# Attention values by column groups of two heads, with rotary, maxima and inverse sums placed elsewhere

## The chip, the core and the metric

One core of a Trainium2 chip runs the whole program in one launch. The metric is the time of an execution in microseconds (us) on the device. TensorE (PE in the rows) multiplies, VectorE is DVE, ScalarE is ACT, GpSimd is POOL, and SyncE (SP) issues the transfers. The engines run their own queues in order and meet at semaphores.

## What is computed

```python
q_rot, k_rot = rotate(q), rotate(k)                # 4 batches x 8 heads, 576 positions, 64 wide
scores = q_rot @ k_rot.T / 8
attn = exp(scores - rowmax(scores)); attn /= attn.sum(-1) + 1e-9
x = concat_heads(attn @ v)                         # 2304 tokens x 512
h = x @ w_in;  x = (h - tanh(h)) @ w_out           # 512 -> 2048 -> 512
h = x @ w_in2; out = (h * sigmoid(1.702 h)) @ w_out2
```

All of it is float32. The kernel keeps that precision in the scores and in the two expert layers by cutting an operand into a high part in the rounded format fp32r and a low rest, and multiplying the parts; probabilities times V is a plain float32 product.

## The kernel before, in words

The first part is attention, head by head, 32 heads in 16 pairs (heads 2p and 2p+1 share the 128 partitions of a load). A head has TILES = 5 tiles of 128 rows; 576 = 4*128 + 64. For each head:

- `load` (line 199) brings k and q transposed, and a copy with the halves exchanged (`turned`); `rope` on VectorE (line 656) turns them with three operations for k and three for q, for a pair at once.
- `keys_hi`, `queries_hi` on ScalarE (lines 547, 553) make the high parts; SyncE copies them to the other half of the partitions (`copy_k`, `copy_q`, lines 217, 221); `keys_lo`, `queries_lo` on VectorE (lines 677, 682) make the low rests. This runs PREPARED = 3 heads ahead in 4 sets of buffers.
- "M" tiles: `near_scores` (line 406) gives scores good enough for the row maxima, with queries on the partitions; `row_max` on VectorE (line 665) reduces each tile to a column. Then "R": `maxima_across` (line 418) transposes the five columns, and `place_maxima` (line 670, VectorE, one operation with a mask) writes them as rows into `q_max`.
- "S" tiles: `scores` (line 423) gives scores minus maxima with keys on the partitions, in four multiplications; `exp` on ScalarE (line 532) writes `probs`; `probs_v` (line 441) multiplies two tiles behind (PV_LAG). Its weights are `v_one`, 64 columns of V beside 64 columns of ones, so that the sums of the probabilities fall out in the other 64 partitions. It makes two multiplications of 288 columns a tile.
- `copy_pv` on ScalarE (line 540) empties the accumulator; the sums go through SyncE to `invert` on VectorE (line 688), through memory and back as `inv_wide`, GpSimd multiplies (`normalise`, line 375), and `store_x` writes the head pair to memory.

M, R and S tiles take turns in three slots of two PSUM banks each, in the order that `ring_order` (line 46) writes out by hand. The tile at place i waits in `slot_free` (line 393) until the reader of the tile at place i-3 is done: `exp` for S, `row_max` for M, `place_maxima` for R.

The second part, two expert layers of 6 units of 384 tokens, runs over 16 slices of the hidden width: `first_product` (line 471), tanh or sigmoid on ScalarE, a product or difference on VectorE, cut again, `second_product` (line 489). Tokens are fetched and cut a unit ahead (`load_x`, `cut_x`, from slice CUT_AT = 8 on); for the first unit this is done during attention (`early_x`), as are the first weights (`early_w`).

Of the kernel before, what the change touches and what calls it, by code (L numbers as in the profile page):

```python
# [40 lines left out]
PROBS = 5  # L41
PV_LAG = 2
PREPARED = 3


def ring_order():

    order = []
    for h in range(-2, NHEADS):
        now, ahead = h >= 0, 0 <= h + 1 < NHEADS  # L50
        for t in range(TILES):
            if now:
                order.append(("S", h, t))
            if ahead and t < 2:
                order += [("M", h + 1, 2 * t + 1), ("M", h + 1, 2 * t + 2)]
            if ahead and t == 2:
                order.append(("R", h + 1, 0))
        if h + 2 < NHEADS:
            order.append(("M", h + 2, 0))
    return order  # L60
# [5 lines left out]
def program(nc, q, k, v, w_in1, w_out1, w_in2, w_out2, cos_t, sin_t, out):  # L66
    q_d, k_d = (t.rearrange("b h d s -> (b h d) s") for t in (q, k))
    v_d = v.rearrange("b h s d -> (b h) s d")
    x_scratch = [nc.dram_tensor(f"x_scratch{m}", [DM, TOKENS], F32, kind="Internal").ap() for m in range(LAYERS)]
    inv_scratch = nc.dram_tensor("inv_scratch", [PAIRS, 2, SEQ], F32, kind="Internal").ap()  # L70
# [3 lines left out]
    with ExitStack() as ctx:  # L74
# [8 lines left out]
        pv_banks = PS[:, 6:8, 0:HALF]  # L83
# [9 lines left out]
        tile_mask = g_raw[0:TILES, :, :].rearrange("p a n -> p (a n)")[:, 0:PADDED].rearrange("p (t n) -> p t n", t=TILES)  # L93
        g_hi = sb("g_hi", [P, STAGES, UNIT], F32R)
        g_lo = sb("g_lo", [P, STAGES, UNIT], F32R)
        y_sb = sb("y_sb", [P, KC, BANK])
        w_parts = [sb(f"w_parts{j}", [P, 4, BANK], F32R) for j in range(APART)]
# [8 lines left out]
        k_one = [sb(f"k_one{j}", [P, PADDED], F32R, one_stack) for j in range(4)]  # L106
        q_hh = [sb(f"q_hh{j}", [P, PADDED], F32R, one_stack) for j in range(4)]
        q_max = [sb(f"q_max{j}", [P, PADDED], F32R, one_stack) for j in range(4)]
        v_one = [sb(f"v_one{j}", [P, 2, TILES, P], stack=one_stack) for j in range(2)]
        probs = [sb(f"probs{j}", [P, SEQ], stack=one_stack) for j in range(PROBS)]  # L110
# [3 lines left out]
        pv_sb = [sb(f"pv_sb{j}", [P, SEQ], stack=one_stack) for j in range(4)]  # L114
        sums = [sb(f"sums{j}", [P, 2 * SEQ // P], stack=one_stack) for j in range(2)]
        inv_wide = [sb(f"inv_wide{j}", [P, SEQ], stack=one_stack) for j in range(2)]
        x_out = [sb(f"x_out{j}", [P, SEQ], stack=one_stack) for j in range(2)]
# [8 lines left out]
        v_ready_to_load = sem("v_ready_to_load")  # L126
# [50 lines left out]
        def slot_columns(slot, cols):  # L177
            return slot.rearrange("p b n -> p (b n)")[:, 0:cols]
# [19 lines left out]
        def _(sp):  # L198
# [85 lines left out]
            for h in range(-1, NHEADS):  # L284
# [19 lines left out]
                if h == 12:  # L304
                    load_x(0, 0)
# [508 lines left out]
```

## Time and profile before

| | |
|---|---|
| median of 3 runs | 1148.81 us (1148.41 to 1148.97) |
| the profiled execution, its own time | 1147.27 us |
| its span in the trace | 1145.5 us, so 1.8 us lie around it |
| mean granted clock of TensorE | 0.997 |
| busy TensorE / VectorE / ScalarE / GpSimd | 1104.1 / 552.4 / 425.7 / 57.1 us |

A matmul's record starts when it is taken up and ends when its last result is modelled to have left, so records overlap: the distance between starts tells what the array needs, the length of a record doesn't. A plain float32 multiplication leaves two records, each with its own weight load; one on fp32r leaves one.

### The profile page before, as it was taken

What the parts mean: (1) busy time and instruction counts of PE and PEld (TensorE: products, weight loads), DVE (VectorE), ACT (ScalarE), POOL (GpSimd) and SP (SyncE); (2) the same over time, 40 slices, a digit from 0 to 9 for tenths busy, and PEclk for the clock granted to TensorE, in tenths of its full rate; (3) what the DMA queues carried; (4) which work ended last, traced back from release to release, by engine and by line L of the source; (5) the groups of instructions that cost most, each with busy time, mean ns of one, the idle gap of its engine ahead of it and who ended that gap; (6) DMA issues with size and microseconds to landing.
All of it is one profiled execution on the core that took longest, in us unless ns stands there. A gap on an engine that the chain in (4) does not pass through costs nothing.

```text
span 1145.5 us, 15078 instructions
## 1 busy us (share of the span) xinstructions
PE 1104.1 (96%) x5952; PEld 1017.8 (89%) x5952; DVE 552.4 (48%) x879; ACT 425.7 (37%) x747; POOL 57.1 (5%) x62
## 2 busy tenths in 40 slices
PE   2999998999999999999999999999999999999998
PEld 1888877787789999999999999999999999999997
DVE  7888887888736433232233333455232322323222
ACT  2555554555544423222222323445232222323222
POOL 3011111102111000000000000000000000000000
PEclk9999999999999999999999999999999999999999
DMA  6355557566315300000000100062000000000000
GB/s 182 95 158 127 155 154 201 136 169 166 87 61 178 102 28 29 28 28 11 19 28 28 29 28 28 1 193 83 28 28 28 28 1 28 28 28 1 28 1 28
DMA packets 78854, 79.85 MB, mean 70 GB/s; under 512 B 30144, under 2 KB 55744, under 8 KB 78784
## 3 DMA queue, kind: packets, MB, share of 16 engines
q1 hardware_dynamic: 78784, 78.89, 24.1%
q8 instruction: 47, 0.77, 0.3%
q14 instruction: 23, 0.19, 0.1%
HBM read 55.12 MB, written 14.23 MB: 61 GB/s over the span
## 4 chain that ended last, share of the span: by engine, by line
PE 89%; DVE 7%; SPq 1%; DMA 1%; POOL 1%; issue 1%; ACT 0%; POOLq 0%; DVEq 0%; ACTq 0%
PE PS L485 35%; PE PS L503 17%; PE PS L500 17%; PE PS L449 10%; PE PS L414 3%; PE PS L431 3%; PE PS L437 3%; DVE neg_max L667 2%; DVE q_max L684 1%; DVE k_hl L679 1%; DVE q_max L674 1%; DMA turned_k<-k_dram 1%; DVE raw_q L662 0%; DVE w_parts L697 0%; DVE raw_q L660 0%
## 5 line engine op out<-in xcount | busy, mean ns | idle before, releaser
L485 PE MATMUL PS<-x_hi,w_parts 128*128 128x384 f32 x1536 | 423.1, 336 | 0.0
L742 DVE TENSOR_TENSOR g_raw<-PS,act_t 128x384 f32<-128x384 f32 x192 | 107.0, 557 | 400.2 <-ACT act_t L610 202.1
L485 PEld LDWEIGHTS PS<-x_hi,w_parts 128*128 128x128 f32 x1536 | 280.5, 188 | 4.3
L485 PE MATMUL PS<-x_lo,w_parts 128*128 128x384 f32 x768 | 257.2, 335 | 0.0
L500 PE MATMUL PS<-g_hi,w_parts 128*128 128x384 f32 x768 | 210.3, 334 | 0.8 <-DVE g_lo L747 0.8
L503 PE MATMUL PS<-w_parts,g_hi 128*128 128x512 f32 x576 | 195.1, 393 | 1.0 <-DVE y_sb L756 0.8
L449 PE MATMUL PS<-probs,v_one 128*128 128x288 f32 x640 | 183.4, 409 | 0.3 <-ACT pv_sb L545 0.3
L747 DVE TENSOR_TENSOR g_lo<-g_raw,g_hi 128x384 fp32r<-128x384 f32 x192 | 107.7, 561 | 113.6 <-ACT g_hi L617 113.6
L537 ACT ACTIVATE probs<-PS 128x576 f32<-128x576 f32 x160 | 104.0, 650 | 129.6 <-PE PS L437 126.3
L485 PEld LDWEIGHTS PS<-x_lo,w_parts 128*128 128x128 f32 x768 | 144.2, 188 | 4.2
L617 ACT ACTIVATE g_hi<-g_raw 128x384 fp32r<-128x384 f32 x192 | 100.8, 525 | 122.9 <-DVE g_raw L742 119.7
L500 PEld LDWEIGHTS PS<-g_hi,w_parts 128*128 128x128 f32 x768 | 140.0, 188 | 1.1 <-DVE g_lo L747 1.1
L449 PEld LDWEIGHTS PS<-probs,v_one 128*128 128x128 f32 x640 | 112.4, 191 | 18.1 <-issue 0.5
L667 DVE TENSOR_REDUCE neg_max<-PS 128x1 f32<-128x576 f32 x160 | 113.8, 746 | 30.1 <-PE PS L414 29.5
L500 PE MATMUL PS<-g_lo,w_parts 128*128 128x384 f32 x384 | 128.3, 334 | 0.0
L503 PEld LDWEIGHTS PS<-w_parts,g_hi 128*128 128x128 f32 x576 | 108.1, 188 | 21.9 <-issue 1.1
L610 ACT ACTIVATE act_t<-PS 128x384 f32<-128x384 f32 x96 | 47.2, 492 | 212.5 <-PE PS L485 212.5
L608 ACT ACTIVATE act_t<-PS 128x384 f32<-128x384 f32 x96 | 47.2, 492 | 206.9 <-PE PS L485 206.9
L414 PE MATMUL PS<-k_hl,q_hh 128*128 128x288 f32 x320 | 86.7, 376 | 34.8 <-DMA q_hh<-q_hh 17.5
L503 PE MATMUL PS<-w_parts,g_lo 128*128 128x512 f32 x288 | 113.7, 395 | 0.0
L414 PEld LDWEIGHTS PS<-k_hl,q_hh 128*128 128x128 f32 x320 | 56.4, 200 | 51.8 <-issue 19.7
L431 PE MATMUL PS<-q_hh,k_hl 128*128 128x288 f32 x320 | 80.0, 332 | 0.0
(51 smaller groups left out, 741.3 us busy)
## 6 DMA issues: line engine op xcount, KB each, us to landing
x_raw<-x_scratch SPq DMA_DIRECT2D x12, 768.0 KB, 4.5
raw_w<-moe_w_in_dram SPq DMA_DIRECT2D x32, 256.0 KB, 3.1
raw_w<-moe_w_out_dram SPq DMA_DIRECT2D x32, 256.0 KB, 3.3
raw_k<-k_dram SPq DMA_DIRECT2D x16, 288.0 KB, 3.5
turned_k<-k_dram SPq DMA_DIRECT2D x64, 72.0 KB, 3.2
raw_q<-q_dram SPq DMA_DIRECT2D x16, 288.0 KB, 3.8
turned_q<-q_dram SPq DMA_DIRECT2D x64, 72.0 KB, 3.5
k_one<-k_hl SPq DMA_DIRECT2D x32, 144.0 KB, 2.4
```

Source lines behind the costliest of these rows:

```text
L414: last = nc.tensor.matmul(slot[:, b, :], q_hh[h % 4][:, t * P:(t + 1) * P], k_hl[h % 4][:, b * HALF:(b + 1) * HALF], start=True, stop=True)
L431: nc.tensor.matmul(slot[:, b, :], k_hl[h % 4][:, keys], q_hh[h % 4][:, b * HALF:(b + 1) * HALF], start=True, stop=False)
L449: last = nc.tensor.matmul(pv_banks[:, b, :], v_one[h // 2 % 2][:, h % 2, t, :], probs[g % PROBS][:, b * HALF:(b + 1) * HALF], start=t == 0 ...
L485: last = nc.tensor.matmul(h_banks[j % 2], w_parts[j][:, w, c * P:(c + 1) * P], x[par][:, c, :], start=(c == 0 and w == 0 and x is x_hi), s ...
L500: last = nc.tensor.matmul(acc_banks[c][:, 0:UNIT], w_parts[j][:, w, c * P:(c + 1) * P], g[:, s, :], start=start, stop=stop)
L503: last = nc.tensor.matmul(acc_banks[c], g[:, s, c * P:(c + 1) * P], w_parts[j][:, w, :], start=start, stop=stop)
L537: nc.scalar.activation(probs[g % PROBS][:, :].rearrange("p (b n) -> p b n", b=2), slot_halves(slot_of("S", h, t)), ACT.Exp).then_inc(exp_d ...
L608: nc.scalar.activation(act_t[:, j % 2, :], h_banks[j % 2], ACT.Tanh).then_inc(act_done, 1)
L617: nc.scalar.activation(g_hi[:, j % STAGES, :], g_raw[:, j % 2, :], ACT.Copy).then_inc(g_hi_done, 1)
L667: nc.vector.tensor_reduce(neg_max[h % 2][:, t:t + 1], slot_halves(slot_of("M", h, t)), AX.XY, ALU.max, negate=True).then_inc(max_done, 1)
L742: nc.vector.tensor_tensor(g_raw[:, j % 2, :], h_banks[j % 2], act_t[:, j % 2, :], ALU.subtract if m == 0 else ALU.mult).then_inc(g_done, 1)
L747: nc.vector.tensor_tensor(g_lo[:, j % STAGES, :], g_raw[:, j % 2, :], g_hi[:, j % STAGES, :].bitcast(F32), ALU.subtract).then_inc(g_lo_don ...
```

## The change

Attention goes pair by pair. A new schedule (`near_plan`, `near_tiles`, `pair_steps`) interleaves the two heads tile by tile, with the ten M tiles of the next pair between. One step of TensorE is: S of the even head; at the fifth step the two transposes R of the next pair; the first M tiles of the step; `values` of the step before; S of the odd head; the second M tiles. `values` replaces `probs_v`: V of the even head stands in the array's columns 0 to 63 and V of the odd head in 64 to 127, each fed by its own probabilities, 512 columns and then 64; the sums are made by four multiplications with 32 columns of ones, one in each quarter of the columns. The other edits: rotary runs on VectorE for pair 0 and from pair 3 on, and on GpSimd for pairs 1 and 2; ScalarE places the maxima, in five operations a head, each with a column of the identity as its scale; there are 6 sets of keys and queries instead of 4; V is laid out by the host in tiles, one transfer a pair; the accumulator is emptied by three copies a pair; GpSimd no longer normalises, the values are stored unscaled, and the inverse sums are fetched a unit at a time and multiplied in by VectorE before the tokens are cut in the first layer (`scale_x`).

```diff
@@ schedule @@
-PROBS = 5
-PV_LAG = 2
-PREPARED = 3
+PROBS = 6
+SETS = 6
+UNITS_PV = PAIRS * TILES
+def near_plan(pair):
+    if pair == 0:
+        return [(0, 0), (0, 2), (2, 2), (2, 2), (0, 0)]
+    return [(1, 2), (1, 2), (1, 2), (1, 0), (0, 0)]
+def near_tiles(pair):
+    return [(2 * pair + i % 2, i // 2) for i in range(2 * TILES)]
 def ring_order():
+    order = [("M", h, t) for h, t in near_tiles(0)] + [("R", 0, 0)]
+    for pair in range(PAIRS):
+        for n, (first, second) in enumerate(pair_steps(pair)):
+            order.append(("S", 2 * pair, n))
+            if n == TILES - 1 and pair + 1 < PAIRS:
+                order.append(("R", 2 * pair + 2, 0))
+            order += [("M", h, t) for h, t in first]
+            order.append(("S", 2 * pair + 1, n))
+            order += [("M", h, t) for h, t in second]
+        def score_count(h, t):
+            return h // 2 * 2 * TILES + 2 * t + h % 2 + 1
-        early_x = {17: (0, 1), 19: (2, 3)}
-        early_w = {21: 0, 23: 1, 25: 2, 27: 3, 31: 4}
+        early_x = {8: (0, 1), 9: (2, 3)}
+        early_w = {10: 0, 11: 1, 12: 2, 13: 3, 15: 4}
@@ SyncE @@
+            def fetch_sums(pair):
+                sp.wait_ge(pv_copied, pair + 1)
...
+                for g in range(4):
+                    sp.dma_start(sums[pair % 2][32 * g:32 * g + 32, :],
+                                 sum_sb[pair % 2][32 * g:32 * g + 1, :].rearrange("o (p j) -> o p j", p=32)).then_inc(sums_in[pair % 2], 16)
+                if m == 0:
...
+                    for a in range(2):
+                        rows = inv_scratch.rearrange("c a n -> a c n")[a:a + 1, :, u * UNIT:(u + 1) * UNIT]
+                        sp.dma_start(inverses[own(a), :, :], rows.broadcast_to([HD, KC, UNIT])).then_inc(inverses_in, 16)
+            for pair in range(PAIRS):
+                if pair:
+                    fetch_sums(pair - 1)
+                    store_x(pair - 1)
+                if pair + 2 < PAIRS:
+                    copy_k(2 * pair + 4)
+                    copy_q(2 * pair + 4)
+                if pair + 1 < PAIRS:
+                    load_v(pair + 1)
+                if pair + 2 < PAIRS:
+                    copy_k(2 * pair + 5)
+                    copy_q(2 * pair + 5)
+                if pair:
+                    store_inverse(pair - 1)
+                if pair + 4 < PAIRS:
+                    for t, src in (("k", k_d), ("q", q_d)):
+                        sp.wait_ge(k_lo_done if t == "k" else q_lo_done, 2 * pair + 6)
+                        load(t, src, pair + 4)
@@ TensorE @@
                 else:
-                    pe.wait_ge(row_done, h + 1)
+                    pe.wait_ge(row_done, h + 2)
-            def probs_v(g):
...
+            def values(unit):
+                pair, t = divmod(unit, TILES)
+                pe.wait_ge(exp_done, 2 * unit + 2)
+                if t == 0:
+                    pe.wait_ge(loaded["v"][pair % 2], pair // 2 * 16 + 16)
+                    if pair:
+                        pe.wait_ge(pv_copied, pair)
+                first, last = t == 0, t == TILES - 1
+                p = [probs[(2 * unit + a) % PROBS] for a in range(2)]
+                for bank, cols in ((values_wide, slice(0, BANK)), (values_tail, slice(BANK, SEQ))):
+                    for a in range(2):
+                        nc.tensor.matmul(bank[own(a), :], v_sb[pair % 2][:, t, own(a)], p[a][:, cols],
+                                         start=first, stop=last, skip_group_check=True)
+                for g in range(4):
+                    done = nc.tensor.matmul(sum_rows[32 * g:32 * g + 32, :], ones[:, t // FULL, :],
+                                            p[g // 2][:, g % 2 * HALF:(g % 2 + 1) * HALF], start=False, stop=last,
+                                            skip_group_check=True)
+                done.then_inc(pv_done, 1)
@@ ScalarE @@
+            def copy_pv(pair):
...
+                nc.scalar.activation(pv_sb[pair % 2][:, 0:BANK], values_wide, ACT.Copy)
+                nc.scalar.activation(pv_sb[pair % 2][:, BANK:SEQ], values_tail, ACT.Copy)
...
+                nc.scalar.activation(sum_sb[pair % 2][:, :], sum_rows, ACT.Copy).then_inc(pv_copied, 1)
+            def place_maxima(h):
+                act.wait_ge(r_ready, h + 1)
+                for t in range(TILES):
+                    last = nc.scalar.activation(q_max[h % SETS][max_rows(h % 2), t * P:(t + 1) * P],
+                                                slot_of("R", h - h % 2)[0:TILES, h % 2, 0:P], ACT.Copy, scale=ident[0:TILES, t:t + 1])
+                last.then_inc(row_done, 1)
+                for n in range(TILES):
+                    exp(2 * pair, n)
+                    if n == 0 and pair:
+                        copy_pv(pair - 1)
+                    if n == TILES - 1 and pair + 1 < PAIRS:
+                        place_maxima(2 * pair + 2)
+                    exp(2 * pair + 1, n)
+                    if n == TILES - 1 and pair + 1 < PAIRS:
+                        place_maxima(2 * pair + 3)
...
+                    elif b < NHEADS:
+                        if n == 1:
+                            keys_hi(a)
+                            queries_hi(a)
+                        if n == 2:
+                            keys_hi(b)
+                        if n == 3:
+                            queries_hi(b)
@@ VectorE, for pairs from 1 on (a, b = 2 * pair + 4, 2 * pair + 5) @@
+                    for h, t in first:
+                        row_max(h, t)
...
+                        if n == 1 and pair + 3 < PAIRS:
+                            rope("k", pair + 3)
+                        if n == 2:
+                            split(a)
+                        if n == 3:
+                            split(b)
+                        if n == 4 and pair + 3 < PAIRS:
+                            rope("q", pair + 3)
+                    if n == 3 and pair:
+                        invert(pair - 1)
+                    for h, t in second:
+                        row_max(h, t)
...
+            def scale_x(u, chunks=range(KC)):
+                dve.wait_ge(x_loaded, u * 16 + 16)
+                dve.wait_ge(inverses_in, u * 32 + 32)
+                for c in chunks:
+                    nc.vector.tensor_tensor(x_raw[:, c, :], x_raw[:, c, :], inverses[:, c, :], ALU.mult).then_inc(x_scaled, 1)
@@ GpSimd @@
-            for pair in range(PAIRS - 1):
-                normalise(pair)
-            normalise(PAIRS - 1)
+            pool.wait_ge(q_lo_done, 2)
+            for pair in (1, 2):
+                rope("k", pair)
+                rope("q", pair)
```

## Rows read from the trace of the kernel before

**Rows 1.** The page: span, busy time of each engine.
```profile
span 1145.5 us, 15078 instructions
PE 1104.1 (96%) x5952; PEld 1017.8 (89%) x5952; DVE 552.4 (48%) x879; ACT 425.7 (37%) x747; POOL 57.1 (5%) x62
```

**Rows 2.** Stretches: start:end length, busy us (records) of PE, PEld, DVE, ACT, POOL, clock, DMA share, GB/s.
```profile
40.00:150.00 110.00, 109.78 (x618) 93.57 (x616) 96.48 (x145) 63.27 (x97) 14.06 (x10) 1.00 0.54 140
150.00:170.00 20.00, 18.15 (x103) 15.20 (x102) 18.11 (x24) 10.17 (x16) 3.77 (x2) 1.00 0.62 166
170.00:190.00 20.00, 17.99 (x102) 15.12 (x101) 15.74 (x21) 10.04 (x16) 3.51 (x2) 1.00 0.74 203
190.00:210.00 20.00, 17.59 (x88) 14.16 (x87) 16.37 (x24) 10.60 (x17) 2.83 (x2) 0.91 0.62 156
210.00:290.00 80.00, 75.76 (x420) 63.78 (x419) 70.90 (x106) 45.37 (x70) 11.51 (x8) 1.00 0.60 160
290.00:310.00 20.00, 17.59 (x91) 14.89 (x90) 14.93 (x19) 9.84 (x16) 3.90 (x2) 0.91 0.32 87
...
400.00:500.00 100.00, 100.00 (x579) 100.00 (x578) 30.53 (x56) 27.84 (x56) 0.00 (x0) 1.00 0.07 24
```

**Rows 3.** The chain between 160 and 180 us, its last piece.
```profile
176.30 6.15 DMA turned_k<-k_dram
```

**Rows 4.** Groups between 95 and 149 us, three head pairs long.
```profile
L449 PE MATMUL PS<-probs,v_one 128*128 128x288 f32 x119 | 33.8, 406 | 0.0
L667 DVE TENSOR_REDUCE neg_max<-PS 128x1 f32<-128x576 f32 x30 | 21.5, 746 | 5.0 <-PE PS L414 4.9
L537 ACT ACTIVATE probs<-PS 128x576 f32<-128x576 f32 x30 | 19.5, 651 | 21.2 <-PE PS L437 20.3
...
L382 POOL TENSOR_TENSOR x_out<-pv_sb,inv_wide 64x576 f32<-64x576 f32 x6 | 8.4, 1405 | 46.2 <-DMA inv_wide<-inv_scratch 46.0
L674 DVE TENSOR_TENSOR q_max<-PS,g_raw 5x640 fp32r<-5x640 f32 x6 | 4.9, 810 | 0.1
```

**Rows 5.** TensorE in order of time, 160 to 163 us: start, length, records.
```profile
160.13 1.14 PE L449 MATMUL PS<-probs,v_one 128*128 128x288 f32 x4
161.10 0.27 PE L421 MATMUL PS<-ident,neg_max 128*5 128x128 f32 x1
161.13 0.51 PE L431 MATMUL PS<-q_hh,k_hl 128*128 128x288 f32 x2
161.48 0.43 PE L437 MATMUL PS<-q_max,k_one 69*128 69x288 f32 x2
161.74 1.13 PE L449 MATMUL PS<-probs,v_one 128*128 128x288 f32 x4
```

**Rows 6.** A multiplication's end and the exponential behind it; ScalarE back to back.
```profile
108.38 0.43 PE L437 MATMUL PS<-q_max,k_one 69*128 69x288 f32 x2
...
108.84 0.65 ACT L537 ACTIVATE probs<-PS 128x576 f32<-128x576 f32 x1
...
257.74 0.63 ACT L537 ACTIVATE probs<-PS 128x576 f32<-128x576 f32 x1
...
258.27 0.67 ACT L557 ACTIVATE q_hh<-raw_q 64x576 fp32r<-64x576 f32 x1
...
258.84 0.63 ACT L537 ACTIVATE probs<-PS 128x576 f32<-128x576 f32 x1
```

**Rows 7.** Groups of ScalarE over the whole span, by width.
```profile
L625 ACT ACTIVATE y_sb<-PS 128x512 f32<-128x512 f32 x10 | 5.4, 596 | 2.2 <-PE PS L503 2.2
L625 ACT ACTIVATE y_sb<-PS 128x384 f32<-128x384 f32 x12 | 5.2, 488 | 2.2 <-PE PS L500 2.2
...
L583 ACT ACTIVATE warm<-ident 128x1 f32<-128x1 f32 x1 | 0.2, 203 | 0.0
```

**Rows 8.** The start: first near scores, first maxima, first transpose, first scores.
```profile
17.46 1.78 PE L414 MATMUL PS<-k_hl,q_hh 128*128 128x288 f32 x6 [17.46 <-DMA q_hh<-q_hh]
...
19.49 3.42 DVE L667 TENSOR_REDUCE neg_max<-PS 128x1 f32<-128x576 f32 x5
...
23.82 0.68 PE L431 MATMUL PS<-q_hh,k_hl 128*128 128x288 f32 x2
```

**Rows 9.** Groups of VectorE in the expert layers.
```profile
L742 DVE TENSOR_TENSOR g_raw<-PS,act_t 128x384 f32<-128x384 f32 x192 | 107.0, 557 | 400.2 <-ACT act_t L610 202.1 <-ACT act_t L608 198.1
...
L703 DVE TENSOR_TENSOR x_lo<-x_raw,x_hi 128x384 fp32r<-128x384 f32 x48 | 23.6, 553 | 0.1
```

More of the change, by code:

```diff
@@ new lines, in _ @@
+            for h in range(2, 4):
+                copy_k(h)
+                copy_q(h)
+            for t, src in (("k", k_d), ("q", q_d)):
+                sp.wait_ge(k_lo_done if t == "k" else q_lo_done, 4)
+                load(t, src, 3)
+            for pair in range(PAIRS):
[13 more added lines that the diff above has]
+                if pair + 4 < PAIRS:
+                    for t, src in (("k", k_d), ("q", q_d)):
+                        sp.wait_ge(k_lo_done if t == "k" else q_lo_done, 2 * pair + 6)
+                        load(t, src, pair + 4)
+                if pair == 6:
@@ new lines, in _ @@
+            maxima_across(0)
+            for pair in range(PAIRS):
+                for n, (first, second) in enumerate(pair_steps(pair)):
+                    scores(2 * pair, n)
+                    if n == TILES - 1 and pair + 1 < PAIRS:
+                        maxima_across(pair + 1)
+                    for h, t in first:
+                        near_scores(h, t)
+                    if pair * TILES + n:
+                        values(pair * TILES + n - 1)
+                    scores(2 * pair + 1, n)
+                    for h, t in second:
+                        near_scores(h, t)
@@ L520, in unit @@
                 second_product(m, u, FC - 1)
[L522 removed]
             first_product(0, 0, 0, 0)
[L524 removed]
+            values(UNITS_PV - 1)
             first_product(0, 0, 0, 1)
@@ L704, in cut_x @@
                                             ALU.subtract).then_inc(x_lo_done, 1)
-            for j in range(4):
+            nc.vector.memset(ones[:, 0, :], 1.0)
+            nc.vector.memset(ones[0:TAIL, 1, :], 1.0)
+            nc.vector.memset(ones[TAIL:P, 1, :], 0.0)
+            for j in range(SETS):
                 dve.wait_ge(cleared, j + 1)
-                last = nc.vector.memset(k_one[j][max_rows(j % 2), :].bitcast(F32), 1.0)
+                last = nc.vector.memset(k_one[j][max_rows(j % 2), 0:SEQ].bitcast(F32), 1.0)
@@ L796, in rope_tables, with value_tiles @@
     return [np.concatenate([t, t], 0) for t in tables]
+def value_tiles(v):
+    t = np.zeros((PAIRS, PADDED, 2, HD), np.float32)
+    t[:, 0:SEQ] = v.reshape(PAIRS, 2, SEQ, HD).transpose(0, 2, 1, 3)
+    return t.reshape(PAIRS, TILES, P, P).transpose(0, 2, 1, 3)
 def kernel(**inputs):
```

409 lines of the change are left out of this document (181 added, 228 removed).

## The prediction, made before the changed kernel ran

> **What bounds the kernel now.** I read the page first: TensorE is busy for 1104.1 of 1145.5 us, VectorE for 552.4 [rows 1]. The share is an average over two parts, so I read stretches next. In the expert layers TensorE has no gap at all and VectorE works 30.5 us of 100 [rows 2]: nothing that the change does there can shorten it, and only the edit on VectorE could lengthen it. In attention TensorE is busy for 109.78 of 110 us between 40 and 150 us, with VectorE at 96.48 and ScalarE at 63.27 [rows 2]. From 150 to 310 us it loses time: 1.85, 2.01 and 2.41 us in three stretches of 20, 4.24 us in the 80 behind them, 2.41 us in the last, together 12.9 us, and twice the granted clock reads 0.91, one dip to the 1.2 GHz level each [rows 2]. The longest single piece is a wait of 6.15 us for a load of keys that stands behind eight transfers of weights on SyncE's queue [rows 3].
>
> The groups between 95 and 149 us give the price of a head pair: 60 probabilities-times-V multiplications in 119 found records (120 are due), 30 maxima and 30 exponentials are three pairs, so a pair takes 54 / 3 = 18.0 us [rows 4].
>
> **What `values` costs on TensorE.** The four records of a tile of `probs_v` last 1.14 us together and one lasts 0.406 [rows 4, 5], so starts are (1.14 - 0.406) / 3 = 0.24 us apart for 288 columns, and a tile costs 0.97 us, a tile of both heads 1.94. A record of 512 columns is then 512 / 288 * 0.242 = 0.43 us, one of 64 columns 0.05. Records double, 16 for 8 a pair tile. No row shows two multiplications in different column groups at once, so I bound it. All one after the other: 4 * 0.43 + 4 * 0.05 + 8 * 0.242 = 3.9 us. Groups fully side by side: 2 * 0.43 + 2 * 0.05 + 2 * 0.242 = 1.45 us. The nearest rows are those of narrow weights between wide ones: the transpose with 5 columns starts at 161.10, exactly four intervals of 0.24 behind 160.13; the second record of L431 must start one interval of 0.13 before L437 at 161.48, so its first one began to stream at about 161.22. The narrow one cost 0.12 us, though its own record is 0.27 long [rows 5]: narrow weights enter and leave with the work around them in flight. That speaks for an array that takes instructions of another column range as it goes, and I take 1.45 us, plus 0.05 for hand-overs (their bound is the 0.15 us by which a record outlasts its interval). That is 1.50 for 1.94, -0.44 us a pair tile, -2.2 us a pair. Without the hand-overs a pair has 18.0 - 2.5 = 15.5 us of TensorE work.
>
> **What the new order adds.** Before, TensorE hardly waits in the steady stretch. To see whether it will, I walk through a pair with durations from rows. S costs 4 * 0.131 = 0.53 us, an M tile 0.26. An exponential starts 0.2 us after its last multiplication stopped streaming, since its record outlasts the interval by 0.16 and 0.03 more pass [rows 6], lasts 0.65 [rows 4], and the waiting multiplication streams about 0.16 later, with its weights still to load.
> (a) Slot of the transposes. The first M tile of a pair stands three places behind R, so it waits until both heads' maxima are placed. From the end of S of the even head's fifth tile TensorE has 0.22 (transposes) + 1.45 + 0.53 + 0.53 = 2.7 us to do. ScalarE can start the odd head's exponential 0.2 us behind that S, at 2.4, issues the five narrow copies behind it at 3.0 and is done at 4.05. ScalarE's 1, 384 and 512 columns last 203, 488 and 596 ns [rows 7], so 128 columns last 0.28; back to back ScalarE starts 0.53 to 0.57 us apart what lasts 0.63 to 0.67 [rows 6], so the narrow ones come every 0.20 us. With 0.16 to restart: a wait of 1.5 us.
> (b) Behind `values` of the old pair ScalarE makes three copies of 512, 64 and 288 columns, 1.0 us, ahead of the exponential of the odd head's first tile. The next S needs that slot: 0.2 + 1.0 + 0.65 + 0.16 = 2.0 us, against 1.05 us of work (S and two M): a wait of 1.0 us.
> (c) At the third and fourth tile, S of the even head needs the slot of the odd head's S before it, with only two M between: 0.2 + 0.65 + 0.16 - 0.53 = 0.5 us, twice.
> (d) An M tile waits for a maximum that stands behind the three operations of the keys' rotary on VectorE, and `values` once for an exponential behind the splitting on ScalarE: 0.4 and 0.3 us.
> Together 4.2 us a pair. A pair takes 15.5 + 4.2 = 19.7 us in place of 18.0: +1.7 * 16 = +27 us, and the hand-overs add 0.05 * 80 = +4.
>
> **What goes.** The 12.9 us of late waits [rows 2]. Copies now run two pairs ahead in 6 sets and loads of keys a pair ahead, so a burst of weights, 6.15 us late at its worst, has some 16 us of cover; the early cutting of tokens and weights falls into time that VectorE now has: 16.7 us a pair before, less two placements of 0.81 [rows 4], is 15 of 19.7. I take all 12.9; without that cover they stay.
>
> **The start.** Ten M tiles must be reduced before the first S instead of five. The first maximum starts 2.03 us behind the first multiplication at 17.46, five take 3.42 us [rows 8], so ten end at about 26.3, and with transposes and placing S starts near 28, not 23.8. Four M tiles of 0.26 are only moved here, and the next pair's are done sooner: net +2 us. GpSimd turns pairs 1 and 2 in 12 operations; its nearest row is 1.4 us for 64 partitions [rows 4], so 17 us, until about 33 us. Pair 1 is asked for at 30, pair 2 much later; up to 4 us of stall here go into the range.
>
> **At nothing.** 32 multiplications of GpSimd (1.4 us each) waited for transfers all the time [rows 4] and nobody near waited for them. SyncE issues 21 transfers a pair where it had 24 (V one for four, sums four for two, no inverses out) and 2 a unit in the first layer. `scale_x` adds four operations of 0.55 us a unit [rows 9] at the ninth slice, so VectorE and, behind it, ScalarE are held for about 4.5 us with the cutting; the next slice's g is then ready some 0.3 us before TensorE asks, and if it isn't, the cost is under 0.5 us for each of five units.
>
> **Sum.** 1147.3 (profiled execution) + 27 + 4 + 2 - 12.9 = 1167. That execution lies 1.5 us below the median of 1148.8, so I forecast 1168 us.
>
> **Rivals.**
> 1. *Short waits, faster.* If (a) to (d) come to less than (16 * 2.5 + 12.9 - 2 - 4) / 16 = 2.9 us a pair, the kernel is faster. The place is ScalarE's queue at the pair change: with narrow copies every 0.1 us, copies of the accumulator in 0.6, and exponentials picked up while M tiles last, (a) is 0.8, (b) 0.6, (c) and (d) 0.7, together 2.1: 1168 - 16 * 2.1 = 1134. For it: in the rows short operations are the least certain, and ScalarE idles 21.2 us before 30 exponentials [rows 4]. Against it: 0.2 us is what one column alone takes.
> 2. *Groups in file.* The two halves of a float32 multiplication use the same columns, so the low half waits for the high one, and if TensorE begins records strictly in order the next group can only run beside the low half. V then takes 3 * 0.43 + 2 * 0.05, the sums 5 * 0.242: 2.6 us, +0.67 on 1.94; waits as before but for (d), 3.7: 1147.3 + 80 * 0.67 + 16 * 3.7 + 2 - 12.9 = 1249, 1251 for the median. For it: every record in the rows starts behind the one ahead of it. The Trainium skill, "TensorE: Matmul & The Clock Gate", The mechanism, says that matmuls keep program order in start and end; the rows agree, and whether a pending half blocks the next group is not in them.
> 3. *No side by side at all.* 3.9 us a pair tile: + 80 * 1.93 instead of 0.67, so 1352. For it: nothing but that no row shows an overlap.
> 4. *Drains.* Each pair tile goes from 128-column weights to 64, to 32 and back. If each passage let the array run empty, 0.16 us by which a record outlasts its interval, it would be 3 * 0.16 * 80 = 38 us: 1168 - 4 + 38 = 1202. The transpose in [rows 5] cost 0.12 us with both its passages, which speaks against it. The Trainium skill, "TensorEngine Tiling (Array Packing)", Key Properties, states that a change of tiling mode drains TensorE; by that rule the sum is this rival's, and the trace disagrees as far as it shows such a change.
>
> **Chances.** Forecast 0.35, rival 1 0.27, rival 2 0.20, rival 3 0.10, rival 4 0.08. A measurement of this kernel tells some 0.2% (2.3 us) from no change. Of rival 1 and of the forecast's lower edge 0.05 fall within it: faster 0.25, same 0.05, slower 0.70. The range goes from 1130 (waits of 2 us a pair) to 1260 (rival 2 with some stalls of the start) and leaves out rival 3 and some edges. The forecast's own range is 1150 to 1190.
>
> **What would show it.** Records of `values`: starts of the two heads' wide multiplications nearly together and a pair tile in 1.5 us (2.6 in file, 3.9 one by one, 1.9 with drains). The distance of pairs 19.7 us with TensorE's waits for the placed maxima (1.5) and for exponentials (1.0, 0.5, 0.5). No wait for keys near 176 us. ScalarE's narrow copies 0.28 us long and 0.20 apart. The expert layers unchanged to 2 us. The forecast is wrong if the pair tile isn't near 1.5 us, or if ScalarE doesn't hold TensorE at the pair change.

## The result, and the profile after

The changed kernel takes 1204.41 us (median of four runs, 1202.62 to 1205.79), the kernel before 1148.66 beside it (1148.41 to 1148.97): ratio 1.048, 95% interval [1.0466, 1.0502]. It is slower by 55.7 us. The forecast was 1168, so sign and range held, but the loss is nearly three times the +19 that was forecast. The profiled execution of the changed kernel took 1203.67 us, 56.4 more than that of before.

The page of the changed kernel, against [rows 1]:

```profile
span 1201.9 us, 16365 instructions
PE 1133.3 (94%) x6592; PEld 959.0 (80%) x6592; DVE 527.8 (44%) x860; ACT 457.0 (38%) x923; POOL 26.1 (2%) x42
```

TensorE stays the busiest, but is now idle for 1201.9 - 1133.3 = 69 us where it was for 41. Stretches of the changed kernel, columns as in [rows 2]:

```profile
40.00:150.00 110.00, 96.09 (x678) 58.07 (x670) 72.57 (x107) 59.97 (x132) 0.00 (x0) 0.95 0.45 112
150.00:310.00 160.00, 141.62 (x991) 82.97 (x990) 108.20 (x164) 89.54 (x195) 0.00 (x0) 0.95 0.56 135
...
450.00:550.00 100.00, 100.00 (x579) 100.00 (x578) 32.30 (x60) 28.07 (x57) 0.00 (x0) 1.00 0.12 35
```

In attention TensorE waits for 13.9 of 110 us where it waited for 0.2; the expert layers are full again. The first multiplication of the experts begins at 390.64 us instead of 337.05, +53.6; the other 2.8 come behind it.

Where the 53.6 lie is read from the transposes, one pair of which stands in every head pair. The distances from one pair's to the next, worked out from their starts:

```
before: 18.3 18.2 18.2 18.2 18.2 18.2 18.2 20.3 24.4 20.1 19.5 19.5 19.5 22.5 18.2
after:  22.3 26.4 21.5 21.5 22.6 21.5 21.5 22.9 22.4 22.3 23.8 24.0 24.0 24.0 24.0
```

Three stages: the first two distances lose 12.2 us, the next five 17.4 (a steady pair takes 21.46 instead of 18.2), the last eight 23.3, although before had its own losses there.

**The pair tile.** TensorE in order of time, the stretch that answers to [rows 5]:

```profile
158.37 0.42 PE L428 MATMUL PS<-k_hl,q_hh 128*128 128x288 f32 x2
158.73 1.19 PE L469 MATMUL PS<-probs,v_sb 128*64 128x512 f32 x8
159.85 0.69 PE L473 MATMUL PS<-probs,ones 128*32 128x288 f32 x8
160.47 0.53 PE L447 MATMUL PS<-g_lo,g_hi 128*128 128x288 f32 x2
```

Eight records with 64 columns of V and eight of ones, then S. The single records of that stretch, start in us and distance to the record ahead in ns:

```
158.503  132  M,    128 columns of weights, 288 streamed
158.726  223  V,    64 columns, 512 streamed, even head, high half
158.733    7  V,    the odd head's
159.206  473  V,    even head, low half
159.212    6  V,    the odd head's
159.636  424  V,    64 streamed, high half (then 6, 49, 6)
159.849  152  ones, 32 columns, 288 streamed (then 7, 6, 8)
160.116  246  ones, low half (then 7, 7, 6)
160.471  335  S,    128 columns, 288 streamed, first record
160.712  241  S,    second record
160.843  131  M-part of S
```

Two things are to be seen. First, the column groups run fully side by side: records of different groups start 6 to 8 ns apart, also where the low halves wait for the high ones. Second, each change of the weights' width leaves a gap. M's last record owes 0.131, V starts 0.092 behind that and its first record takes 0.473 + 0.007 where 0.427 would do: 0.145 us for 128 to 64 columns. By the same working, always from a group's record to its own next one, 64 to 32 costs 0.13 (0.105, and 0.027 in the first record), and 32 to 128 costs 0.22 (0.115 before S's first record, 0.11 within it). Together 0.50 us. A pair tile takes 158.634 to 160.581, 1.95 us, and took 1.94: the columns saved 0.49 and the passages took 0.50. The expectations below were written with 0.12 to 0.20 a passage and 0.46 a tile, which leaves out part of the 7 ns steps between groups.

Two more readings tell what kind of gap this is. Where S stood still for an exponential, its first two records start at 174.908 and 175.146, 0.24 us apart as behind the sums, and not 0.13 as elsewhere: behind a passage TensorE starts up as it does behind a wait. And the change between float32 and fp32r isn't the cause: in the kernel before, V is followed by S at one width, V's last record at 98.895 and S's second at 99.270, which is 0.375 us for the 0.242 + 0.131 that they owe. The length of such a pair of records says nothing of a gap, since the first is taken up early; in the kernel before, S directly behind V is

```profile
162.50 0.64 PE L431 MATMUL PS<-q_hh,k_hl 128*128 128x288 f32 x2
```

**The pair change.** The timeline of ScalarE, with TensorE beside it, where the next pair's maxima are placed:

```profile
183.09 0.38 PE L437 MATMUL PS<-ident,neg_max 128*5 128x128 f32 x2
...
184.14 0.65 ACT L561 ACTIVATE probs<-PS 128x576 f32<-128x576 f32 x1
...
184.82 1.36 ACT L578 ACTIVATE q_max<-PS,ident 5x128 fp32r<-5x128 f32 x5
...
186.20 0.65 ACT L561 ACTIVATE y_sb<-PS 128x576 f32<-128x576 f32 x1
...
186.32 0.50 PE L453 MATMUL PS<-q_max,k_one 69*128 69x288 f32 x2
...
186.75 1.34 ACT L578 ACTIVATE q_max<-PS,ident 5x128 fp32r<-5x128 f32 x5
187.99 0.62 ACT L561 ACTIVATE y_sb<-PS 128x576 f32<-128x576 f32 x1
...
188.14 0.53 PE L428 MATMUL PS<-g_hi,g_lo 128*128 128x288 f32 x2 [1.32 <-ACT q_max L578]
```

The transposes are made at 183.1, their slot is free at 188.1: the ten narrow copies take 1.36 and 1.34 us and each set stands behind an exponential. The waits between 97 and 183 us, four pairs long (total, times, longest):

```profile
PEld PS L469 <- issue: 14.0, 55, 0.5
PEld PS L447 <- issue: 7.9, 16, 0.9
...
PE PS L428 <- ACT q_max L578: 5.3, 4, 1.3
PEld PS L447 <- ACT y_sb L561: 4.6, 10, 0.7
PEld PS L447 <- ACT probs L561: 3.1, 6, 0.7
```

Against the list of the prediction, per pair and measured from end of stream to next start: (a) 1.58 us (said 1.5), (b) 0.70 (1.0), (c) 0.48 twice (0.5 twice), (d) nothing (0.7), and 0.29 for the first S, which waits for its own placed maxima (not foreseen). Together 3.5 us, where 4.2 were forecast.

**The late pairs.** Stretches at and behind one pair change of the changed kernel, columns as in [rows 2]:

```profile
252.00:257.00 5.00, 2.82 (x24) 1.72 (x20) 3.88 (x8) 4.95 (x15) 0.00 (x0) 0.99 0.60 65
257.00:260.40 3.40, 3.40 (x18) 1.08 (x17) 0.76 (x1) 0.04 (x1) 0.00 (x0) 0.51 0.99 288
```

At the change ScalarE is full (4.95 of 5 us) and TensorE half idle (2.82 of 5); right behind it the granted clock is 0.51, the 1.2 GHz level, for 3.4 us, in which up to 1.7 us of work are lost. ScalarE's queue at such a change:

```profile
274.84 0.68 ACT L602 ACTIVATE q_hh<-raw_q 64x576 fp32r<-64x576 f32 x1
275.54 1.06 ACT L618 ACTIVATE w_parts<-raw_w 128x1024 fp32r<-128x1024 f32 x1
276.51 0.64 ACT L561 ACTIVATE probs<-PS 128x576 f32<-128x576 f32 x1
277.17 1.35 ACT L578 ACTIVATE q_max<-PS,ident 5x128 fp32r<-5x128 f32 x5
```

The cutting of expert weights (1.06 us) now stands ahead of the exponential and the maxima. From the eleventh distance on a pair takes 23.8 to 24.0 us: 21.46, some 0.8 of more waiting (the tenth distance, which has no dip, takes 22.3), and up to 1.7 of clock. There are nine such dips in attention, the first of them, at 55.5 us, twice as long as the others; before had two.

**The start.** The 26.4 us at the second distance are one wait of 4.4 us: TensorE's first M tile of pair 2 starts at 55.98. GpSimd was long done (its last rotary operation starts at 33.52 and lasts 1.80). ScalarE's and SyncE's rows show who was late:

```profile
51.67 1.34 ACT L578 ACTIVATE q_max<-PS,ident 5x128 fp32r<-5x128 f32 x5
52.91 0.67 ACT L602 ACTIVATE g_lo<-raw_q 64x576 fp32r<-64x576 f32 x1
...
53.60 0.47 SPq L242 DMA_DIRECT2D g_lo<-g_lo  x1
...
55.98 0.82 PE L428 MATMUL PS<-g_hi,g_lo 128*128 128x288 f32 x2 [4.37 <-issue]
```

The queries' high part is cut behind the narrow copies, then copied by a transfer that is issued at 53.60 and that the multiplication needs. The narrow copies are not all of it: with the maxima on VectorE (a run below) TensorE still waits 3.1 us there, until 57.73. The cut of the queries then stands behind an exponential that itself waits for its scores until 54.11.

**The expert layers.** TensorE where the first ones begin:

```profile
398.02 0.44 PE L525 MATMUL PS<-g_hi,w_parts 128*128 128x384 f32 x1 [0.95 <-DVE g_lo L844]
...
437.19 0.44 PE L525 MATMUL PS<-g_hi,w_parts 128*128 128x384 f32 x1 [0.98 <-DVE g_lo L844]
```

One gap of 0.95 us at the hand-over from attention, one of 0.98 behind the ninth slice with `scale_x` in it, and one of 0.20: 2.1 us, where before had a single gap of 0.78 at its hand-over. Another 1.1 of the +2.8 is attention's: its last pair tile, with both heads, stands behind the experts' first slice and takes up 2.0 us there, where before had one head's, 0.9. The rest is in small pieces.

### The profile page after: what moved, and what is told of

Its sections match the earlier page's. It is cut to its first block, busy times and chain, and to the rows that moved or that the text cites. A ratio compares the mean times of both kernels' runs of the same rounds, so it can differ in the third digit from the quotient of the medians.

```text
span 1201.9 us, 16365 instructions
## 1 busy us (share of the span) xinstructions
PE 1133.3 (94%) x6592; PEld 959.0 (80%) x6592; DVE 527.8 (44%) x860; ACT 457.0 (38%) x923; POOL 26.1 (2%) x42
## 4 chain that ended last, share of the span: by engine, by line
PE 84%; ACT 8%; issue 3%; DVE 3%; POOL 1%; DMA 0%; SPq 0%; ACTq 0%; POOLq 0%; DVEq 0%
PE PS L510 33%; PE PS L528 16%; PE PS L525 16%; PE PS L469 7%; PE PS L447 4%; PE PS L473 4%; ACT q_max L578 3%; PE PS L453 2%; ACT y_sb L561 2%; PE PS L428 2%; ACT probs L561 1%; DVE neg_max L736 1%; ACT q_hh L602 1%; ACT w_parts L618 1%; POOL q_max L386 0%
## 5 line engine op out<-in xcount | busy, mean ns | idle before, releaser
L561 ACT ACTIVATE y_sb<-PS 128x576 f32<-128x576 f32 x79 | 51.1, 649 | 76.8 <-PE PS L453 76.5
L453 PE MATMUL PS<-q_max,k_one 69*128 69x288 f32 (+1 forms) x320 | 71.2, 305 | 6.7 <-ACT q_max L578 6.3
L428 PE MATMUL PS<-k_hl,q_hh 128*128 128x288 f32 x220 | 46.8, 325 | 30.9 <-DMA q_hh<-q_hh 17.9
L469 PE MATMUL PS<-probs,v_sb 128*64 128x512 f32 (+1 forms) x324 | 71.6, 455 | 0.8 <-ACT probs L561 0.6
L525 PEld LDWEIGHTS PS<-g_lo,w_parts 128*128 128x128 f32 x384 | 72.1, 188 | 0.0
L561 ACT ACTIVATE probs<-PS 128x576 f32<-128x576 f32 x81 | 52.1, 645 | 46.6 <-PE PS L453 46.3
```

The costliest lines, as they stand in the source:

```text
L428: last = nc.tensor.matmul(slot[:, b, :], q_hh[h % SETS][:, t * P:(t + 1) * P], k_hl[h % SETS][:, b * HALF:(b + 1) * HALF], start=True, sto ...
L453: last = nc.tensor.matmul(slot[:, b, :], k_one[h % SETS][rows, keys], q_max[h % SETS][rows, b * HALF:(b + 1) * HALF], start=False, stop=True)
L469: nc.tensor.matmul(bank[own(a), :], v_sb[pair % 2][:, t, own(a)], p[a][:, cols], start=first, stop=last, skip_group_check=True)
L525: last = nc.tensor.matmul(acc_banks[c][:, 0:UNIT], w_parts[j][:, w, c * P:(c + 1) * P], g[:, s, :], start=start, stop=stop)
L561: nc.scalar.activation(probs[i % PROBS].rearrange("p (b n) -> p b n", b=2), slot_halves(slot_of("S", h, t)), ACT.Exp).then_inc(exp_done, 1)
```

## The experiments

Two theories. **Passages:** every change of the weights' width costs TensorE 0.12 to 0.22 us, which cancels what the column groups save. **Queue:** ScalarE's queue at the pair change is what holds TensorE, and the narrow copies are what makes it long. Against each stands that it is only a mark of something else: of the records' count, of the order of the steps, of late data.

**An added passage.** The sums are made between the wide and the narrow V multiplications, same operations in another order, so 64, 32, 64 and back instead of 64, 32 and back.

```diff
-                for bank, cols in ((values_wide, slice(0, BANK)), (values_tail, slice(BANK, SEQ))):
+                for part, (bank, cols) in enumerate(((values_wide, slice(0, BANK)), (values_tail, slice(BANK, SEQ)))):
+                    if part and not first:
+                        sum_products(p, t, last)
```

> The four multiplications of the sums stand between V's wide and V's narrow pair instead of behind both, in every pair tile but the first of a pair: no work and no wait more, one more passage between weights of 64 and of 32 columns in 64 pair tiles. Theory (each passage lets the array run empty, 0.12 to 0.20 us by the trace): +0.12 to +0.15 us in 64 tiles, about +9 us on 1204.4, so 1213 us, and a fourth gap in each tile. Rival (the three gaps of a tile belong to semaphore waits or to the change between fp32r and float32): no gap more, 1204 us within 2.

Measured: 1211.0 us, 1.054 [1.0521, 1.0559], 6.6 over the changed kernel. Its trace, in order of time:

```profile
207.68 0.59 PE L478 MATMUL PS<-probs,v_sb 128*64 128x512 f32 x1
...
208.21 0.44 PE L459 MATMUL PS<-probs,ones 128*32 128x288 f32 x2
...
208.83 0.27 PE L478 MATMUL PS<-probs,v_sb 128*64 128x64 f32 x1
...
209.09 0.53 PE L447 MATMUL PS<-q_hh,k_hl 128*128 128x288 f32 x2
```

A fourth gap appears, between 32 and 64 columns, and such a tile takes 0.15 us more. The steady pair grows by 0.40 us, not by 0.60 (four of its five tiles have the new order), mostly because the wait for placed maxima shrinks from 0.29 to 0.13. So the passages are real and cost time; the work is otherwise the same.

**One width.** V of both heads as 128 columns, no sums but for the first tile.

```diff
-                        nc.tensor.matmul(bank[own(a), :], v_sb[pair % 2][:, t, own(a)], p[a][:, cols],
+                        nc.tensor.matmul(bank, v_sb[pair % 2][:, t, :], p[a][:, cols],
...
+                if unit == 0:
+                    for g in range(4):
```

> V of both heads is loaded as 128 columns of weights for either head's probabilities, so that the two heads go one behind the other through the whole array; the sums are left out but in the very first pair tile. The output is not attention's: rows of the two heads mix and the sums are stale. Streaming is 4 * 0.43 + 4 * 0.05 = 1.94 us a pair tile where side by side it is 1.45. Theory (passages cost 0.46 us a tile): they vanish, so 1.94 against 1.45 + 0.46 = 1.91, and the time stays at 1204 us within 5. Rival (the gaps belong to the waits): they stay, 2.40 us a tile, 80 * 0.49 = +39 us, 1243 us.

Measured: 1216.02 us, 1.0591 [1.0575, 1.0607], +11.6. The gaps between widths are gone, but a tile takes 2.16 us, not 1.94. TensorE in order of time:

```profile
144.02 2.38 PE L469 MATMUL PS<-y_sb,v_sb 128*128 128x512 f32 x8
146.20 0.51 PE L447 MATMUL PS<-q_hh,k_hl 128*128 128x288 f32 x2
```

Its eight single records start 0.429 us apart while 512 columns are streamed and 0.11 where 64 are, twice the 0.053 that they took with 64 columns of weights: my reading is that with a full set of weights for 64 streamed columns the load is the longer of the two, but nothing tests it. Both my prices missed this; four of these records cost 0.22 us a tile more. The run shows the gaps go with the change of width, but not its price.

**No sums.** The sums' four multiplications a tile left out but for the first tile: what is left has one passage to 64 columns and one back.

> The multiplications that make the sums are left out but in the very first pair tile; V stays side by side in 64-column groups. The inverse sums are stale. Theory: a tile loses 0.48 us of streaming and one passage of 0.12, 0.60 * 80 = 48 us, of which some comes back since exponentials are then late by more: a walk through the queues gives -37 us, 1167 us; a tile 1.31 us. Rival (sums are hidden behind the waits for exponentials): under -10 us, over 1194.

Measured: 1174.72 us, 1.023, -29.7. A pair without a dip takes 19.46 us, 2.0 less. A tile is 0.62 us shorter (0.48 of columns, 0.14 of passages), so 3.1 should go, and waits took 1.1 of it back. The trace has 13 stretches at the 1.2 GHz level, four more than the changed kernel, and a mean clock of 0.975. TensorE is idle for a larger share of each pair here, and the clock gives back part of the gain.

**Maxima on VectorE.** The changed kernel with the old placing: one VectorE operation a head against a mask, in place of ScalarE's five.

```diff
-                for t in range(TILES):
-                    last = nc.scalar.activation(q_max[h % SETS][max_rows(h % 2), t * P:(t + 1) * P],
-                                                slot_of("R", h - h % 2)[0:TILES, h % 2, 0:P], ACT.Copy, scale=ident[0:TILES, t:t + 1])
+                nc.vector.tensor_tensor(q_max[h % SETS][max_rows(h % 2), :].rearrange("p (t n) -> p t n", t=TILES), rows,
+                                        tile_mask, ALU.mult).then_inc(row_done, 1)
```

> Maxima are placed by VectorE again, one operation of 0.81 us a head with a mask, ahead of the rotary of the queries; ScalarE's ten narrow copies a pair are gone. Theory (ScalarE's queue holds the slot of the transposes for 1.6 us a pair and the first S for 0.3): both waits nearly vanish, some 1.6 us in 15 pairs = -24 us, and with shorter gaps fewer dips of the clock, up to 10 us more: 1170 to 1181 us. Rival (VectorE takes as long there, or the wait goes on to the exponentials): over 1198 us.

Measured: 1176.63 us, 1.0248 [1.0233, 1.0263], -27.8. Stretches:

```profile
40.00:150.00 110.00, 100.87 (x713) 60.01 (x712) 84.95 (x124) 49.20 (x85) 0.00 (x0) 0.95 0.48 115
150.00:310.00 160.00, 150.16 (x1106) 90.29 (x1107) 133.08 (x198) 81.88 (x141) 0.00 (x0) 1.00 0.60 143
```

From 150 us on the clock is 1.00 and a pair takes 20.43 us, the late ones at most 20.9. The wait for the slot of the transposes is 0.52 instead of 1.58. This edit alone is half of the whole loss: 1.0 us a pair in the steady stretch, and 3.3 in the last five pairs, where a dip each went with it.

**Rotary on VectorE.** Pairs 1 and 2 turned by VectorE instead of GpSimd, in the changed kernel.

```diff
-            pool.wait_ge(q_lo_done, 2)
-            for pair in (1, 2):
-                rope("k", pair)
-                rope("q", pair)
```

> The changed kernel with the rotary of pairs 1 and 2 on VectorE too, behind the first two splits and in the steps of pair 0. Theory (GpSimd turns pair 2 too late, its first near scores wait 4.8 us at 51 us and the clock dips for 6.8 us behind it): that wait goes, 5 to 8 us less, 1197 to 1199 us. Rival (VectorE, which also reduces and splits, makes them wait as long): 1204 us within 2.

Measured: 1205.19 us, 1.0497 [1.0483, 1.0511]: no gain. The waits between 50 and 60 us:

```profile
PE PS L413 <- issue: 4.4, 1, 4.4
DVE q_max L742 <- ACT g_lo L587: 2.6, 1, 2.6
```

The long wait stays as it was, and SyncE issues the copy of the queries' high part at 55.97 us, behind ScalarE. GpSimd's rotary costs nothing here.

**The order.** Maxima and rotary on VectorE, and S of the odd head directly behind S of the even one, with the next pair's M tiles shared out by another plan.

```diff
-    return [(1, 2), (1, 2), (1, 2), (1, 0), (0, 0)]
+    return [(1, 2), (2, 1), (2, 1), (1, 0), (0, 0)]
...
+                    scores(2 * pair + 1, n)
```

> Maxima and all rotary on VectorE as in two earlier runs, and another order: values behind the S of the odd head instead of ahead of it, near scores as (1,2), (2,1), (2,1), (1,0), (0,0), and the accumulator copied behind the odd head's first exponential. Theory (what is left of the waits is exponentials that the next S needs too early, 2.5 us a pair): a walk through the queues gives 0.9 us a pair less than with the old order, 14 us, and the rotary's 5 to 8: 1155 to 1158 us from 1176.6. It stays above 1148, since the passages still eat what the column groups save. Rival (the waits only move to the slots of near scores): over 1168 us.

Measured: 1156.68 us (1155.38 to 1158.09), 1.0072 [1.006, 1.0085]. The pair takes 19.36 to 19.40 us from the third distance to the last. Waits between 97 and 174 us:

```profile
PEld PS L418 <- DVE neg_max L714: 4.0, 12, 0.4
...
PEld PS L459 <- ACT probs L551: 0.5, 3, 0.2
PEld PS L459 <- ACT y_sb L551: 0.2, 1, 0.2
```

Of waits for ScalarE 0.7 us are left in four pairs, all ahead of V; the 4.0 us are weights of M tiles that wait for VectorE's maxima. What was left of (a) to (c) went with this edit, 20 us. It is a bundle, though: the order, the plan of M tiles, the place of the accumulator's copies and the rotary were not run one by one here, and the rotary was run alone only where ScalarE still placed the maxima.

**Maxima on ScalarE in the kernel before.** Only that part of the change, alone.

```diff
-            def place_maxima(h):
-
-                dve.wait_ge(r_ready, h + 1)
...
+                for t in range(TILES):
+                    last = nc.scalar.activation(q_max[h % 4][max_rows(h % 2), t * P:(t + 1) * P],
```

> The kernel before with one part of the change alone: ScalarE places the maxima in five narrow copies a head, behind the fourth exponential, and VectorE's operation of 0.81 us a head is gone. Theory (from 150 us on VectorE is the engine that is late in the kernel before, by 1.6 us a pair of cut weights and tokens; ScalarE has room and the slot of the transpose isn't asked for until 3 us later): 3 to 9 us less, about 1143 us. Rival (ScalarE's 1.36 us in a block make the next exponentials late, as in the changed kernel): 1149 us or more.

Measured: 1177.56 us, 1.0254 [1.024, 1.0268], +29. My theory had it as a gain, since VectorE is freed: it fell. A pair takes 20.45 us instead of 18.2. Waits between 95 and 149 us:

```profile
DVE k_hl L681 <- ACT k_hl L558: 7.8, 5, 1.6
...
PE PS L414 <- DVE neg_max L676: 5.2, 5, 1.2
...
DVE q_max L686 <- ACT q_hh L564: 2.6, 5, 0.6
```

ScalarE's copies delay its cutting of keys and queries (one set of five starts at 106.30 us, and the keys behind it are cut at 107.67), VectorE waits for that, and the next maximum stands behind it in VectorE's queue, and the near scores behind the maximum. The work left VectorE and the wait came back by way of it.

**Loads of weights spread, in the kernel before.** One of the bursts behind which [rows 3] waited is issued a part a head.

```diff
-                if h == 14:
-                    for c in range(STAGING):
-                        load_w(0, c)
+                if 14 <= h < 14 + STAGING:
+                    load_w(0, h - 14)
```

> The kernel before with the first eight transfers of weights issued two a head over four heads instead of in one block. Theory (the block makes the loads of keys at 176 us late by 6.15 us, of which TensorE waits 2 to 4): 3 to 5 us less, 1144 us. Rival (VectorE is late there anyway): 1148 us within 1.5.

Measured: 1144.66 us (1143.82 to 1146.19), 0.9967 [0.9955, 0.998], -4.2 us. The pair that took 24.4 us takes 20.3. It is faster than both kernels, and it prices the long wait of before: 4 us of the 6.15.

**V in quarters.** The changed kernel with V in four groups of 32 columns, the width of the sums: one passage fewer a tile, eight records more.

```diff
-                    for a in range(2):
-                        nc.tensor.matmul(bank[own(a), :], v_sb[pair % 2][:, t, own(a)], p[a][:, cols],
+                    for g in range(4):
+                        quarter = slice(32 * g, 32 * g + 32)
+                        nc.tensor.matmul(bank[quarter, :], v_sb[pair % 2][:, t, quarter], p[g // 2][:, cols],
```

> The changed kernel with V taken in four groups of 32 columns instead of two of 64, so that V and the sums have the same column width and a pair tile has two passages instead of three. It issues 8 records more a tile, 6 ns apart in the trace. Theory (a passage costs what it costs whatever stands around it): the gap of 0.118 us between V and the sums goes, 0.12 * 80 = 9 us, of which a third may come back in waits for exponentials: 1195 to 1199 us. Rival (the gap is V's last results leaving before other weights come, or the records more take its place): 1204 us within 2.

Measured: 1192.71 us (1189.5 to 1198.38), 1.0407 [1.0382, 1.0432], -11.7 (-10.1 if each kernel is taken against the kernel before beside it, 1147.08 us here). A tile is 0.15 us shorter: the 0.13 between V and the sums is gone, and V's first record is 0.03 shorter. The steady pair takes 20.90 us, 0.56 less and not 0.77, since the wait for placed maxima grows by 0.16. TensorE in order of time:

```profile
142.75 1.18 PE L470 MATMUL PS<-probs,v_sb 128*32 128x512 f32 x16
143.75 0.67 PE L474 MATMUL PS<-probs,ones 128*32 128x288 f32 x8
144.34 0.53 PE L447 MATMUL PS<-g_lo,g_hi 128*128 128x288 f32 x2
```

Sixteen records of V last as long as eight did (1.18 for 1.19), so the number of records is not what costs.

**Quarters with the order of above.**

> V in four groups of 32 columns on top of the kernel with the other order (maxima and rotary on VectorE, values behind the odd head's S), which took 1156.7 us. Theory: 7 to 9 us less, 1148 to 1150 us, level with the kernel before. Rival as in the run beside it: 1157 us within 2.

Measured: 1146.11 us (1144.93 to 1147.45) against 1147.08 of the kernel before beside it, 0.9995 [0.9986, 1.0004]: -10.6 on the run with the order alone (-8.8 each against its own before), level with before. A pair takes 18.64 to 18.74 us. This is the idea of the change with its avoidable costs taken out, and it gains nothing yet: two passages a tile (some 0.34 us, 27 us in all) still stand against 39 us of columns.

**Another plan of M tiles on top.** `[(1, 1), (1, 1), (3, 0), (3, 0), (0, 0)]` for the pairs behind the first.

> As the run before it, and the near scores spread as (1,1), (1,1), (3,0), (3,0), (0,0). Theory: a walk through the queues puts 0.3 us a pair less of waits than with (1,2), (2,1), (2,1), (1,0), so 4 to 5 us less than the run before it, 1144 to 1146 us: below the kernel before, since its late waits of 12.9 us are gone too. Rival (three near scores in a row wait for their maxima on VectorE): the same or slower than the run before it.

Measured: 1148.32 us, 1.0009 [0.9999, 1.0018], no gain, 2 us over the one above. The steady pair is 0.05 shorter (18.62), but the first two distances together are 0.4 longer, and the ninth to the twelfth (19.3, 18.9, 18.8, 18.8) 1.0.

## Why the prediction was right in its sign and wrong in its size

1. **The pair tile: wrong, and this is the step that failed.** The text had: "narrow weights enter and leave with the work around them in flight", so 1.45 plus 0.05 for hand-overs. Column groups side by side were right (6 to 8 ns apart), and rivals 2 and 3, in file and one by one (2.6 and 3.9 us a tile), are out. But the passages cost 0.50 us, not 0.05: 1.95 for 1.50, +0.45 in each of 80 tiles, 36 us. The added passage and the quarters (+0.15 and -0.15 a tile, with nothing else changed in it) show them as the cause. It is rival 4's mechanism at rival 4's price (3 * 0.16 = 0.48), to which I gave 0.08. That its sum of 1202 us comes so near to 1204 is in part luck: it has the late waits some 10 us and the start and the experts some 7 us too low, and the growth of the pairs (66 us for 49) some 17 us too high. The Trainium skill, "TensorEngine Tiling (Array Packing)", Key Properties, says that a changed tiling mode drains TensorE; that case went by the rule, and the trace of after agrees with it, at 0.13 to 0.22 us a change. The row from which I argued, the transpose with 5 columns between wide weights, was too weak a witness. Of its 0.12 us 0.05 are its own 128 columns, so its two passages cost some 0.07, less than any of these; I stretched that to weights of 64 and 32 columns, three passages for 0.05. The S behind the transpose is no witness either way. Its two records last 0.51 us for the usual 0.43, but behind V, where no width changes and nothing is lost, they last 0.64: the first record is merely taken up early. Why the transposes pass more cheaply is open.
2. **The waits: right in place, nearly in size.** 3.5 us a pair for 4.2. ScalarE's ten narrow copies at 0.27 us each (1.36 for five; said 0.20 apart and 0.28 long, measured 0.25 apart and 343 ns long) bring (a) to 1.58. Rival 1, short waits, is out.
3. **A pair: 19.95 forecast, 21.46 measured.** 19.7 plus 0.25 of hand-overs; the tile adds 2.2 and the waits take 0.7 off. On the pair of before this is +3.26, since that one takes 18.2 and not the 18.0 taken from counts.
4. **The late waits: wrong.** "I take all 12.9." The wait for keys did go, yet the last eight distances of after lie 15.6 us over 21.46 each, where those of before lie 18.4 over 18.2: 3 us gained, not 13. ScalarE's cutting of weights stands in the queue that now sets the pair (0.8 a pair), and the idle time at the pair change is followed by a 3.4 us stretch at the 1.2 GHz level (up to 1.7 a pair; the one dip in the steady stretch cost 1.15). With the maxima on VectorE both nearly vanish (late pairs 20.4 to 20.9). What of the late loss is the clock's alone was not separated.
5. **The start: too low.** +2 forecast; the first two distances lose 12.2 us, 5.7 more than two steady pairs do, and the named risk, GpSimd's rotary, was not it: the wait stays without it. The queries' high part is late in ScalarE's queue, with a transfer behind it. Taking the narrow copies out of that queue leaves 3.1 of the 4.4 us, and in every run of this kernel and its variants the first two distances stay 4 to 8 us over two steady pairs; this loss was not removed.
6. **The expert layers: about right**, 2.8 us with "under 0.5 for each of five units" allowed, but not in that way: the ninth slice of the first unit costs 0.98 once and no other unit anything, and 1.1 is attention's last tile.

The account, on profiled executions: 15 distances at +3.26 make 48.9; the first two add 5.7, a dip in the fifth 1.2, the late ones give back 2.8; the start and the last pair add 0.6, the experts 2.8: 56.4. In terms of parts: the maxima on ScalarE cost 28 us in the changed kernel and 29 in the old one, the order with what was bundled to it 20, the passage between V and sums 9 to 12.

## What to carry to other kernels

Before narrow weights are packed side by side, count the changes of width: each cost 0.12 to 0.22 us here, with 64, 288 or 512 columns streamed around it, so the packed stretch must save more than its passages, and everything packed should have one width. Work moved off an engine that is not the bound is dear when it lands in a queue that a slot or a later stage waits for: look who stands behind it, not how busy its engine is. A short idle stretch at every step of a loop can cost twice, by its own length and by the lower clock behind it.

## What was not expected of the hardware

- A change of weight width costs by direction: to fewer columns 0.145 us from 128 to 64, 0.13 from 64 to 32 and 0.12 from 128 to 32 (V in quarters), to more columns 0.17 from 32 to 64 (the added passage), 0.21 from 64 to 128 (no sums) and 0.22 from 32 to 128. Why they differ is open; with V and sums both 32 wide the passage between them is gone.
- Two float32 multiplications in two column groups start 6 to 7 ns apart, and the high halves of both run ahead of the low halves although one multiplication's two records would stand one behind the other in file. The Trainium skill, "TensorE: Matmul & The Clock Gate", Measured speedup vs the span model, tells of about 4 ns for each further tile; the rows here have 6 to 8.
- A float32 record that streams 64 columns takes 0.053 us with 64 columns of weights and 0.11 with 128.
- The clock fell to the 1.2 GHz level in the midst of attention, for 3.4 us at a time, in the late pairs behind stretches of 5 us in which TensorE was busy for 2.8. In the steady stretch the same pair change passed without a dip four times of five; with 19.4 us pairs whose idle time is spread it fell once. The kernel without sums, with less work between the same waits, fell 13 times; that it does so is shown, what share of its time hangs on it is not.
